# VectorE's inverse root of the next batch moved behind two steps on v, in a three-stage fp32 kernel

## The chip, the cores and the metric

One core of a Trainium2 chip. The metric is the device time of one execution in microseconds: the median was 791.29 over three runs (790.93 to 792.1). The profile is one further execution, of 791.45 us.

## The reference

Batch 8, sequence S = 576, width 512, inner width 1024. Three stages follow each other (einsum and matmul in fp32):

```python
kv  = einsum('bhsd,bhse->bhde', k, v);  out = einsum('bhsd,bhde->bhse', q, kv)
x   = out / sqrt(mean(out * out, -1) + 1e-6) * g_norm          # stage 1: attention, norm
h   = maximum(x @ w_in, 0);  u, v = h[..., :512], h[..., 512:]
v_n = (v - mean(v)) / sqrt(var(v) + 1e-6)                      # stage 2: along the last axis
x   = (u * (w_spatial @ v_n + b_spatial)) @ w_out
h   = maximum(x @ moe2_w_in, 0)                                # stage 3
out = (h * sigmoid(conv3(h))) @ moe2_w_out                     # conv3: three taps along S
```

## The kernel before, in words

Every matrix product of fp32 data is made of three products of parts: an operand is split into a high part (rounded by ScalarE) and a low part (the difference, by VectorE), and high-high, high-low and low-high are summed. This holds for x, for v and for the weights. The product w_out @ moe2_w_in is formed once at the start, so that stage 3 takes the gated values themselves.

**First half (up to about 409 us).** TensorE, ScalarE and VectorE each run body(b) for the 8 batches. Batch b does stage 2 and, for all but the last batch ("ahead"), the attention of batch b + 1. Each engine's order of instructions is written out by hand; engines meet only through counting semaphores (wait_ge). Batches 0 to 2 are unrolled on ScalarE and VectorE, the others run in a loop.

TensorE's order in body(b): kv_product(b + 1) (L404); v_product for the tiles of v (L477), in the order of V_TILES = [0, 1, 2, 4, 3], so that the fifth position is tile 3 and the fourth position is the rest of 64 rows; between them the attention products of b + 1; square_sum(b + 1) (L430), which sums squares over each head; u_product in four parts (L451, 96 matmuls); spatial_product in four parts (L451, 112 matmuls). spatial_product(b, 0) waits for s_vlo to reach 5 (b + 1), that is, for all five v_lo of this batch, and for the first relu of u. kv_product of the next batch waits for `s_g >= b * MT - 1` with the new b and MT = 4: three of the four gates of the batch before.

VectorE's order in body(b): kv_copy(b + 1); then for each position i of the five: v_stats (L1090 to L1097: mean and variance), at the fifth position mean_square(b + 1) (L1041) and inverse_root(b + 1) (L1051 to L1059: one reciprocal and one Newton step on 128 x 144 elements); v_lo of the position before (L1119, for the rest L1121); v_normalise (L1103 to L1112: a reciprocal and a Newton step on one element per row, then the scaling of the tile). After the loop: in batch 0 the low part of the bias row (L1141), v_lo of the fifth position, in batches 1 and 2 the low part of half of w_out2 (L1084), gate(0) (L1126), x_scale(b + 1) four times (L1071), gate(1), x_lo(b + 1) four times (L1076) and once for the rest (L1079), gate(2), gate(3), and four differences of gated blocks (L1174).

ScalarE, in turn, does the relus (L715, L718, L720 for v; L744 for u), the high parts of v (L731; L733 and L734 for the rest), the roots (L694 for r, L725 for v), squares and copies. In batch 0 it also splits w_sp (L853), whose low parts GpSimd forms (L391, L394). In batches 1 and 2 it loads half of w_out2 (L804) and stores its split form to HBM (L812).

SyncE's queue carries most DMAs. In its loop for b: the loads of k, v and q of batch b + 2; spread_r(b + 1), which waits for s_r (set by L1059), stores r0 to HBM in four DMAs (L253), waits for them, and loads it back, each row to 64 partitions, in two DMAs (L258) into rB, called sq_then_r in the profile. x_scale waits for both. Then store_gated(b), which waits for the gates.

**Second half.** Stage 3, batch by batch; nothing of it is touched.

Of the kernel before, what the change touches and what calls it, by code (L numbers as in the profile page):

```python
# [80 lines left out]
def build(nc, q_T, kv_main_dram, kv_rest_dram, consts, w_in, w_sp_T, b_sp, w_out_T, w_in2, w_out2, wo2_dram, op_dram, r_dram, out):  # L81
    with ExitStack() as ctx:
# [940 lines left out]
        def _(dve):  # L1023
# [3 lines left out]
            def kv_copy(a):  # L1027
                dve.wait_ge(s_kv, a + 1)
                dve.wait_ge(s_o, a * MT)
                for half in (0, 1):  # L1030
                    last = dve.tensor_copy(kvd[half * D:(half + 1) * D, :, 1, :],
                                           PS[D:P, KV_BANK, 0:MT * D].rearrange("p (m e) -> p m e", m=MT))
                last.then_inc(s_kvd1, 1)
# [5 lines left out]
            def mean_square(a):  # L1039
                dve.wait_ge(s_ssq, a + 1)  # L1040
                dve.tensor_scalar(ms[:, :], PS[:, ssq_bank(a), 0:QS], 1.0 / D, EPS,  # L1041
                                  ALU.mult, ALU.add).then_inc(s_ms, 1)

            def inverse_root(a):

                dve.wait_ge(s_std, a + 1)
                if isinstance(a, int) and a == 1:
                    dve.wait_ge(s_rP, MT)
                if not isinstance(a, int) or a > 1:
                    dve.wait_ge(s_rst, (a - 1) * 4 * DMA)  # L1050
                dve.reciprocal(r0[:, :], std[:, :]).then_inc(s_nr, 1)  # L1051
                dve.wait_ge(s_nr, a * 4 + 1)
                dve.tensor_tensor(std[:, :], r0[:, :], r0[:, :], ALU.mult).then_inc(s_nr, 1)
                dve.wait_ge(s_nr, a * 4 + 2)
                dve.tensor_tensor(std[:, :], std[:, :], ms[:, :], ALU.mult).then_inc(s_nr, 1)
                dve.wait_ge(s_nr, a * 4 + 3)
                dve.tensor_scalar(std[:, :], std[:, :], -0.5, 1.5, ALU.mult, ALU.add).then_inc(s_nr, 1)
                dve.wait_ge(s_nr, a * 4 + 4)
                dve.tensor_tensor(r0[:, :], r0[:, :], std[:, :], ALU.mult).then_inc(s_r, 1)  # L1059
# [22 lines left out]
            def wo2_low(h, f):  # L1082
                dve.wait_ge(s_wo2_hi, h * MT + f + 1)
                dve.tensor_tensor(wo2_lo[:, f, :], wo2_raw[:, f, :], wo2_hi[:, f, :].bitcast(F32), ALU.subtract).then_inc(s_wo2, 1)  # L1084

            def v_stats(b, p):
                n = P if V_TILES[p] < FULL else REST
                if n == REST:
                    dve.wait_ge(s_vtmp, b + 1)
                    dve.tensor_tensor(v_sb[p % 2][0:n, :], PS[0:n, V_BANK[FULL], 0:F1], v_rest, ALU.add).then_inc(s_vsum, 1)  # L1090
                dve.wait_ge(s_vr, b * NT + p + 1)
                dve.bn_stats(stats[0:n, :], v_sb[p % 2][0:n, :]).then_inc(s_vst, 1)  # L1092
                dve.wait_ge(s_vst, (b * NT + p) * 2 + 1)
                dve.tensor_copy(carrier[0:n, :], stats[0:n, 1:2])
                dve.bn_aggr(mv[0:n, :], stats[0:n, :]).then_inc(s_vst, 1)
                dve.wait_ge(s_vst, (b * NT + p) * 2 + 2)
                dve.tensor_scalar(ve[0:n, :], mv[0:n, 1:2], EPS, None, ALU.add).then_inc(s_ve, 1)  # L1097

            def v_normalise(b, p):
                n = P if V_TILES[p] < FULL else REST  # L1100
                c = (b * NT + p) * 4
                dve.wait_ge(s_vsd, b * NT + p + 1)
                dve.reciprocal(vr0[0:n, :], vsd[0:n, :]).then_inc(s_vrs, 1)  # L1103
                dve.wait_ge(s_vrs, c + 1)
                dve.scalar_tensor_tensor(out=vrr[0:n, :], in0=vr0[0:n, :], scalar=ve[0:n, :], in1=vr0[0:n, :],  # L1105
                                         op0=ALU.mult, op1=ALU.mult).then_inc(s_vrs, 1)
                dve.wait_ge(s_vrs, c + 2)
                dve.tensor_scalar(vrf[0:n, :], vrr[0:n, :], -0.5, 1.5, ALU.mult, ALU.add).then_inc(s_vrs, 1)
                dve.wait_ge(s_vrs, c + 3)
                dve.tensor_tensor(vrs[0:n, :], vr0[0:n, :], vrf[0:n, :], ALU.mult).then_inc(s_vrs, 1)  # L1110
                dve.wait_ge(s_vrs, c + 4)
                dve.tensor_scalar(v_sb[p % 2][0:n, :], v_sb[p % 2][0:n, :], mv[0:n, 0:1], vrs[0:n, :],  # L1112
                                  ALU.subtract, ALU.mult).then_inc(s_vn, 1)

            def v_lo(b, p):
                i, v = V_TILES[p], v_sb[p % 2]
                dve.wait_ge(s_vhi, b * NT + p + 1)
                if i < FULL:
                    dve.tensor_tensor(vn[:, LO, i, :], v, vn[:, HI, i, :].bitcast(F32), ALU.subtract).then_inc(s_vlo, 1)  # L1119
                else:  # L1120
                    dve.tensor_tensor(vnA[REST:P, :], v[0:REST, :], vnA[0:REST, :].bitcast(F32), ALU.subtract).then_inc(s_vlo, 1)  # L1121

            def gate(b, m):
                dve.wait_ge(s_ur, b * MT + m + 1)
                dve.wait_ge(s_sp, b * MT + m + 1)
                dve.tensor_tensor(whole(u_sb[m]), pair[GATE_PAIR[m]], whole(u_sb[m]), ALU.mult).then_inc(s_g, 1)  # L1126

            def body(b, ahead):
                if ahead:
                    kv_copy(b + 1)  # L1130
                for i in range(NT):
                    v_stats(b, i)
                    if ahead and i == NT - 1:
                        mean_square(b + 1)
                        inverse_root(b + 1)
                    if i:
                        v_lo(b, i - 1)
                    v_normalise(b, i)
                if isinstance(b, int) and b == 0:
                    dve.wait_ge(s_b_hi, 1)  # L1140
                    dve.tensor_tensor(wspB[96:97, :], b_raw[96:97, :], wspB[96:97, :].bitcast(F32),  # L1141
                                      ALU.subtract).then_inc(s_b, 1)
                v_lo(b, NT - 1)
                if isinstance(b, int) and b in (1, 2):
                    for f in range(MT):
                        wo2_low(b - 1, f)
                if not ahead:
                    combine_weights()
                gate(b, 0)
                if ahead:  # L1150
                    for m in range(MT):
                        x_scale(b + 1, m)
                gate(b, 1)
                if ahead:
                    for m in range(MT):
                        x_lo(b + 1, m)
                else:
                    for k in range(3):
                        operand_lo(0, k)
                gate(b, 2)  # L1160
                if not ahead:
                    operand_lo(0, 3)
                    operand_lo(0, 4)
                gate(b, 3)
                if ahead:
                    t_a(b)
                    t_b(b)
                    t_c(b)
                else:
                    operand_lo(0, 5)  # L1170
                    operand_lo(0, 6)
# [4 lines left out]
            def t_a(b):  # L1176
                dve.wait_ge(s_To, DMA * b)
                dve.wait_ge(s_g, b * MT + MT)
                t_block(T1, gated(0, 1), gated(0, 0))
                t_block(T3, gated(1, 1), gated(0, 1))  # L1180
# [14 lines left out]
            def combine_weights():  # L1195
                a11, a21, a12, a22 = W[:, 0, 0], W[:, 0, 1], W[:, 1, 0], W[:, 1, 1]
                dve.wait_ge(s_To, DMA * (B - 1))
                dve.tensor_tensor(s_raw[0], a21, a22, ALU.add).then_inc(s_S, 1)
                dve.wait_ge(s_S, 1)
                dve.tensor_tensor(s_raw[1], s_raw[0], a11, ALU.subtract).then_inc(s_S, 1)  # L1200
                weight_lo(S1, 1)
                weight_lo(S2, 2)
                dve.wait_ge(s_Slo, 1)
                dve.tensor_tensor(s_raw[0], a12, s_raw[1], ALU.subtract).then_inc(s_S, 1)
                dve.wait_ge(s_Slo, 2)
                dve.wait_ge(s_S, 3)
                dve.tensor_tensor(s_raw[1], a11, a21, ALU.subtract).then_inc(s_S, 1)
                weight_lo(S4, 3)
                weight_lo(S3, 4)
                weight_lo(A11, 5)  # L1210
                weight_lo(A12, 6)
                weight_lo(A22, 7)
# [240 lines left out]
```

## Time and profile before

| | |
|---|---|
| median of three runs | 791.29 us (790.93 to 792.1) |
| the profiled execution | 791.45 us, its span 789.4 us |
| granted TensorE clock | 1.00 over the span |
| busy: TensorE | 780.9 us (99%) |
| busy: VectorE | 584.9 us (74%) |
| busy: ScalarE | 421.6 us (53%) |
| busy: GpSimd | 29.5 us (4%) |
| GpSimd's last instruction | from 65.96 to 67.45 us |

In the profile PE is TensorE's matmul, PEld its weight load, DVE VectorE, ACT ScalarE, POOL GpSimd and SP SyncE; SPq and ACTq are the DMA issues of a queue. L1059 is line 1059 of the kernel. A wait for several semaphores is put down to whatever ended last, which need not be the one that the code names.

### The profile page before, as it was taken

The numbers are of one execution on the slowest core, as the hardware profiler recorded it, in microseconds if no ns is written. First come the engines' busy times: TensorE is split into PE (matmuls) and PEld (weight loads), VectorE is DVE, ScalarE is ACT, GpSimd is POOL, SyncE is SP. The second block draws the span as 40 slices with busy tenths as digits, with TensorE's granted clock in tenths as the row PEclk, the third lists the DMA queues.
The fourth block names the chain that finished last, engine by engine and source line by source line (L and its number), as shares of the span: only waits on it lengthen the run. The fifth ranks groups of instructions, "written<-read, shape, count | busy, mean of one in ns | idle before, by whom it ended". The sixth has DMA issues, their size and how long they took to land.

```text
span 789.4 us, 15393 instructions
## 1 busy us (share of the span) xinstructions
PE 780.9 (99%) x5654; PEld 701.4 (89%) x5654; DVE 584.9 (74%) x1262; ACT 421.6 (53%) x753; POOL 29.5 (4%) x40
## 2 busy tenths in 40 slices
PE   8999999999999999999999999999999999999997
PEld 7679889797988979899999898998989899898986
DVE  3766786776577475666899989497985979679791
ACT  4664462634335253352557767365774757567562
POOL 4342000000000000000000000000000000000000
PEclk9999999999999999999999999999999999999999
DMA  9872455756334272222192212221021312102102
GB/s 329 301 253 62 172 196 185 293 182 234 96 110 174 75 269 61 105 52 77 39 360 67 103 54 106 67 96 64 4 104 65 105 53 94 64 13 105 53 0 66
DMA packets 35001, 96.86 MB, mean 123 GB/s; under 512 B 2738, under 2 KB 9106, under 8 KB 30228
## 3 DMA queue, kind: packets, MB, share of 16 engines
q1 hardware_dynamic: 33476, 90.09, 33.3%
q10 hardware_dynamic: 1488, 6.30, 2.1%
q8 instruction: 20, 0.33, 0.2%
q14 instruction: 17, 0.14, 0.1%
HBM read 66.11 MB, written 30.28 MB: 122 GB/s over the span
## 4 chain that ended last, share of the span: by engine, by line
PE 93%; DVE 3%; DMA 1%; ACT 1%; issue 1%; SPq 1%; ACTq 0%; DVEq 0%
PE ps L451 27%; PE ps L634 25%; PE ps L626 21%; PE ps L477 11%; PE ps L420 2%; PE ps L404 2%; PE ps L484 2%; PE ps L556 1%; DMA work<-w_out_T_dram 1%; PE ps L430 1%; DVE h_and_sums L1272 0%; DVE vrr L1105 0%; DVE t_then_s L1174 0%; PE ps L544 0%; DVE work L1112 0%
## 5 line engine op out<-in xcount | busy, mean ns | idle before, releaser
L634 PE MATMUL ps<-w_in_split,v_hg_split 128*128 128x512 f32 x832 | 194.9, 389 | 0.0
L634 PEld LDWEIGHTS ps<-w_in_split,v_hg_split 128*128 128x128 f32 x832 | 155.7, 188 | 32.3
L451 PE MATMUL ps<-w_sp_split,v_hg_split 128*128 128x288 f32 x896 | 120.2, 295 | 1.7 <-ACT work L744 1.7
L451 PEld LDWEIGHTS ps<-w_sp_split,v_hg_split 128*128 128x128 f32 x896 | 119.2, 188 | 1.9 <-issue 1.9
L451 PE MATMUL ps<-x_operand_split,w_in_split 128*128 128x288 f32 x768 | 103.8, 295 | 0.0
L451 PEld LDWEIGHTS ps<-x_operand_split,w_in_split 128*128 128x128 f32 x768 | 102.0, 188 | 1.7 <-issue 1.6
L477 PE MATMUL ps<-w_in_split,x_operand_split 128*128 128x512 f32 x384 | 92.8, 394 | 0.0
L477 PEld LDWEIGHTS ps<-w_in_split,x_operand_split 128*128 128x128 f32 x384 | 70.9, 188 | 18.2 <-issue 3.1
L1272 DVE TENSOR_TENSOR h_and_sums<-h_and_sums,ps 128x288 f32<-128x288 f32 x160 | 68.8, 453 | 7.5 <-PE ps L626 7.2
L1126 DVE TENSOR_TENSOR work<-ps,work 128x576 f32<-128x576 f32 x32 | 24.1, 757 | 61.2 <-PE ps L451 60.9
L1272 DVE TENSOR_TENSOR h_and_sums<-work,ps 128x288 f32<-128x288 f32 x64 | 28.3, 452 | 46.8 <-PE ps L626 46.3
L626 PE MATMUL ps<-x_operand_split,w_combined 128*128 128x288 f32 x384 | 61.5, 295 | 0.0
L915 ACT ACTIVATE h_and_sums<-h_and_sums 128x576 f32<-128x576 f32 x64 | 43.4, 678 | 29.3 <-DVE h_and_sums L1272 28.3
L626 PE MATMUL ps<-operand_more_split,w_combined_more 128*128 128x288 f32 x384 | 56.5, 295 | 0.3 <-DVE h_and_sums L1272 0.3
L626 PEld LDWEIGHTS ps<-x_operand_split,w_combined 128*128 128x128 f32 x384 | 54.7, 188 | 0.0
L626 PEld LDWEIGHTS ps<-operand_more_split,w_combined_more 128*128 128x128 f32 x384 | 52.9, 188 | 0.6 <-DVE h_and_sums L1272 0.6
L1315 DVE SCALAR_TENSOR_TENSOR work<-h_and_sums,const_cols,work 128x576 f32<-128x576 f32 x64 | 52.5, 821 | 0.3
L1309 DVE SCALAR_TENSOR_TENSOR work<-h_and_sums,const_cols,work 128x576 f32<-128x576 f32 x64 | 52.5, 820 | 0.0
L921 ACT ACTIVATE work<-h_and_sums,const_cols 128x576 f32<-128x576 f32 x64 | 49.7, 776 | 3.0
L1320 DVE TENSOR_TENSOR work<-h_and_sums,work 128x576 f32<-128x576 f32 x64 | 48.7, 761 | 0.3 <-ACT work L931 0.3
L1092 DVE BATCH_NORM_STATS2 bn_stats<-work 128x6 f32<-128x512 f32 (+1 forms) x40 | 27.5, 688 | 24.1 <-ACT work L715 18.5
L931 ACT ACTIVATE work<-work 128x576 f32<-128x576 f32 x64 | 43.6, 681 | 2.3 <-DVE work L1315 1.8
(124 smaller groups left out, 1037.5 us busy)
## 6 DMA issues: line engine op xcount, KB each, us to landing
kv_raw<-kv_main_dram SPq DMA_DIRECT2D x8, 2048.0 KB, 10.1
q_raw<-q_T_dram SPq DMA_DIRECT2D x8, 1152.0 KB, 7.2
operand_scratch<-t_then_s SPq DMA_DIRECT2D x8, 1152.0 KB, 5.3
operand_raw<-operand_scratch SPq DMA_DIRECT2D x8, 1152.0 KB, 5.5
sq_then_r<-r_scratch SPq DMA_DIRECT2D x14, 576.0 KB, 6.1
operand_scratch<-work SPq DMA_DIRECT2D x24, 288.0 KB, 2.6
operand_more_raw<-operand_scratch SPq DMA_DIRECT2D x8, 864.0 KB, 7.4
w_out_split_scratch<-v_hg_split ACTq DMA_DIRECT2D x2, 2048.0 KB, 8.4
```

The source lines that it names most:

```text
L451: last = pe.matmul(pair[bank][:, c, :], st, mo[:, c * HALF:(c + 1) * HALF], start=(n == 0), stop=(n == len(steps) - 1))
L477: last = pe.matmul(PS[:, V_BANK[i], 0:F1], XG[:, a, m, i * P:(i + 1) * P], WA[:, w, m, F1:2 * F1], start=(n == 0), stop=(n == len(steps) - 1))
L626: last = pe.matmul(PS[:, n % 8, 0:HALF], st, mo, start=(i == 0), stop=(i == len(steps) - 1))
L634: last = pe.matmul(PS[:, ROW_BANK[i], :], x, wout2[:, w, F_ORDER[e], :], start=(e == 0 and n == 0), stop=(e == FT - 1 and n == len(PASSES) ...
L915: act.activation(h_sb[f][:, 1:S + 1], h_sb[f][:, 1:S + 1], ACT.Relu).then_inc(s_hr, 1)
L921: act.activation(t_sb[e % 2], h_sb[f][:, 1:S + 1], ACT.Copy, scale=cols[:, FT + f:FT + f + 1]).then_inc(s_t0, 1)
L931: act.activation(p_sb[e % 2], t_sb[e % 2], ACT.Sigmoid).then_inc(s_sig, 1)
L1092: dve.bn_stats(stats[0:n, :], v_sb[p % 2][0:n, :]).then_inc(s_vst, 1)
L1272: dve.tensor_tensor(dst, x, PS[:, (g * NPROD + k) % 8, 0:HALF], ALU.add).then_inc(s_sum, 1)
L1309: dve.scalar_tensor_tensor(out=t, in0=h_sb[f][:, 0:S], scalar=cols[:, f:f + 1], in1=t, op0=ALU.mult, op1=ALU.add).then_inc(s_cv1, 1)
L1315: dve.scalar_tensor_tensor(out=t, in0=h_sb[f][:, 2:S + 2], scalar=cols[:, 2 * FT + f:2 * FT + f + 1], in1=t, op0=ALU.mult, op1=ALU.add).th ...
L1320: dve.tensor_tensor(p_sb[e % 2], h_sb[F_ORDER[e]][:, 1:S + 1], p_sb[e % 2], ALU.mult).then_inc(s_mul, 1)
```

## The change

On VectorE, in the loop over the five positions, mean_square(b + 1) stays where it is, and inverse_root(b + 1) moves behind the loop, that is, behind v_lo of the fourth position and v_normalise of the fifth. In batch 0 it stands ahead of L1141, in all of them ahead of v_lo of the fifth position.

```diff
                     v_stats(b, i)
                     if ahead and i == NT - 1:
                         mean_square(b + 1)
-                        inverse_root(b + 1)
                     if i:
                         v_lo(b, i - 1)
                     v_normalise(b, i)
+                if ahead:
+                    inverse_root(b + 1)
                 if isinstance(b, int) and b == 0:
                     dve.wait_ge(s_b_hi, 1)
```

## Rows read from the trace of the kernel before

**Rows 1.** The page: busy us (share of the span) and instructions of each engine.

```profile
PE 780.9 (99%) x5654; PEld 701.4 (89%) x5654; DVE 584.9 (74%) x1262; ACT 421.6 (53%) x753; POOL 29.5 (4%) x40
```

**Rows 2.** Timeline of VectorE, end of batch 0: start, duration, instruction [idle before <- releaser].

```profile
62.26 0.30 DVE L1041 TENSOR_SCALAR ms<-ps 128x144 f32<-128x144 f32 x1
63.28 1.05 DVE L1051 RECIPROCAL r<-std 128x144 f32<-128x144 f32 x1 [0.72 <-ACT std L694]
...
64.75 1.42 DVE L1055 TENSOR_TENSOR std<-std,ms 128x144 f32<-128x144 f32 x1
66.19 1.35 DVE L1057 TENSOR_SCALAR std<-std 128x144 f32<-128x144 f32 x1
67.58 0.31 DVE L1059 TENSOR_TENSOR r<-r,std 128x144 f32<-128x144 f32 x1
...
69.47 0.55 DVE L1112 TENSOR_SCALAR work<-work,mean_var,vrs 128x512 f32<-128x512 f32 x1
70.05 0.76 DVE L1141 TENSOR_TENSOR w_sp_split<-w_sp_raw,w_sp_split 1x576 fp32r<-1x576 f32 x1
70.84 0.69 DVE L1119 TENSOR_TENSOR v_hg_split<-work,v_hg_split 128x512 fp32r<-128x512 f32 x1
```

**Rows 3.** Timeline of ScalarE and of GpSimd, the same stretch.

```profile
61.84 0.62 ACT L734 ACTIVATE v_hg_split<-work 64x512 fp32r<-64x512 f32 x1
...
63.15 0.19 ACT L725 ACTIVATE vsd<-ve 128x1 f32<-128x1 f32 x1
...
63.11 1.44 POOL L391 TENSOR_TENSOR w_sp_split<-w_sp_raw,w_sp_split 128x576 fp32r<-128x576 f32 x1 [2.80 <-ACT w_sp_split L853]
64.53 1.47 POOL L391 TENSOR_TENSOR w_sp_split<-w_sp_raw,w_sp_split 128x576 fp32r<-128x576 f32 x1
65.96 1.49 POOL L394 TENSOR_TENSOR w_sp_split<-w_sp_raw,w_sp_split 64x576 fp32r<-64x576 f32 x1
```

**Rows 4.** Timeline of VectorE and of GpSimd, 58 to 60 us.

```profile
59.13 1.20 DVE L1105 SCALAR_TENSOR_TENSOR vrr<-vr,ve 64x1 f32<-64x1 f32 x1
...
58.43 1.88 POOL L391 TENSOR_TENSOR w_sp_split<-w_sp_raw,w_sp_split 128x576 fp32r<-128x576 f32 x1 [3.54 <-ACT w_sp_split L853]
```

**Rows 5.** Timeline of TensorE and VectorE, 71 to 89 us.

```profile
71.79 15.09 PE L451 MATMUL ps<-w_sp_split,v_hg_split 128*128 128x288 f32 x112 [1.67 <-ACT work L744]
86.81 2.55 PE L404 MATMUL ps<-kv_raw 128*64 128x64 f32 x80
...
78.54 3.01 DVE L1071 SCALAR_TENSOR_TENSOR o_x<-o_x,const_cols,sq_then_r 128x576 f32<-128x576 f32 x4 [1.93 <-DMA sq_then_r<-r_scratch]
...
85.13 0.75 DVE L1126 TENSOR_TENSOR work<-ps,work 128x576 f32<-128x576 f32 x1
```

**Rows 6.** The same in batch 1, 109 to 136 us.

```profile
109.86 1.05 DVE L1051 RECIPROCAL r<-std 128x144 f32<-128x144 f32 x1 [0.39 <-ACT std L694]
...
111.90 0.31 DVE L1059 TENSOR_TENSOR r<-r,std 128x144 f32<-128x144 f32 x1
...
123.57 3.00 DVE L1071 SCALAR_TENSOR_TENSOR o_x<-o_x,const_cols,sq_then_r 128x576 f32<-128x576 f32 x4
...
130.32 0.76 DVE L1126 TENSOR_TENSOR work<-ps,work 128x576 f32<-128x576 f32 x1
...
133.85 2.55 PE L404 MATMUL ps<-kv_raw 128*64 128x64 f32 x80
```

**Rows 7.** The store's issue; then queues' packets, MB, share: 121 to 121.5, 104 to 106.

```profile
119.11 0.35 ACTq L812 DMA_DIRECT2D w_out_split_scratch<-v_hg_split  x1
...
q10 hardware_dynamic: 8, 0.13, 81.7%
q1 hardware_dynamic: 13, 0.05, 46.3%
...
q1 hardware_dynamic: 81, 0.71, 86.7%
q10 hardware_dynamic: 85, 0.14, 20.7%
```

## The prediction, made before the change was run

> **What bounds the kernel now.** I read the page's busy shares first: TensorE is busy for 780.9 of 789.4 us [rows 1], so the change can only matter where TensorE waits, or where it could begin to. Next the chain of waits in order of time. It runs over TensorE nearly without a break from 72 us to the end of the first stage (409 us), but from 51 to 71.8 us it runs over VectorE. So I looked at TensorE's own timeline: before the spatial product of batch 0 it stands still for 1.67 us, up to 71.79 [rows 5]. The profile names ScalarE's L744 as releaser. By the code that product waits for the first relu only, which ended long before, and for all five s_vlo, the last from VectorE's L1119, which ends at 71.53 [rows 2]. So VectorE is the cause, and TensorE resumes 0.26 us behind it. Batches 1 to 6 have no such wait, and batch 7 does not pass through the moved call. What the change can win is therefore at most 1.67 us; what it can lose has to be looked for behind the thing that it delays, r.
>
> **The change, part by part.**
>
> *Nothing is added or removed; five instructions move.* inverse_root(b + 1) (L1051 to L1059) goes behind v_lo of position 3 and v_normalise of position 4. It does not go behind v_lo of position 4, the one that TensorE waits for. VectorE still issues all of it, and L1141 too, before that last v_lo. So the text of the change doesn't shorten the list of work ahead of the critical instruction; it can gain only the idle time that the order fills. That is 0.72 us before L1051, the wait for the root [rows 2].
>
> *Batch 0, up to r.* L1041 ends at 62.56 [rows 2]. v_lo(3) has its input at 62.46 [rows 3], so it runs from 62.59 to 63.28 (0.69, as L1119 in rows 2). The root of the variance is there at 63.34 [rows 3], so v_normalise(4) starts at 63.38. Undisturbed, v_lo(3) and v_normalise(4) take 2.13 us together (67.89 to 70.02 in rows 2), 1.4 for the latter. But now it meets GpSimd, whose three operations lie back to back from 63.11 to 67.45 [rows 3]. In the trace those hold VectorE up: L1055 takes 1.42 and ends 0.17 after the second, L1057 takes 1.35 and ends 0.09 after the third [rows 2, 3]; undisturbed the whole inverse root takes 2.35 (109.86 to 112.21 in rows 6), here 4.61. L1105, an instruction of v_normalise on one element, was held in the same way at 59.13: 1.20 us, until GpSimd's end at 60.31 [rows 4]. So the stall isn't a property of the inverse root, and moves onto what takes its place: L1103 (it reads a single tensor, as L1051, which ran beside GpSimd in its usual 1.05) ends at 63.54; L1105 is held to 64.57; L1108 is free, to 64.76; L1110 is held to 66.02; L1112 is held to 67.45 and then needs 0.40 more (its 0.55 less the 0.15 that L1057 saved of its own by having been queued), to 67.85. Then the inverse root runs undisturbed, 2.35: r is there at 70.23 instead of 67.89, **2.34 later**. L1141 (0.76) and the last v_lo (0.69) follow, to 71.74 instead of 71.53: **TensorE resumes 0.21 later**, and the 0.72 is not won. Bounds for this step: if nothing of v_normalise is held, it ends at 64.8, the inverse root meets the third GpSimd operation once and r comes at 68.23 (+0.34); the last v_lo then ends at 69.7 and the whole 1.67 goes. If L1108 is held too, everything is 0.2 later. I take the middle case, since rows 4 show the very instruction held and rows 2 the two kinds that follow.
>
> *Batch 0, behind r.* SyncE's queue waits for r, stores it (four DMAs), waits for them and loads rB (two DMAs); no other call is moved past, and store_gated behind it in that queue waits for later gates anyway. From r to rB it is 10.61 us: 67.89 to 78.50, where VectorE's L1071 has stood idle for the DMA for 1.93 us already [rows 5]. That wait has no cover left, so the 2.34 go straight through. On VectorE, in order, behind L1071 are gate(1), x_lo, gate(2). gate(2), the L1126 at 85.13, ends at 85.88; it will end at 88.22. TensorE's kv_product of the next batch waits for that gate (s_g of 4b - 1). It started at 86.81 [rows 5], with 0.93 to spare. The new start is 88.22 and a hand-over of 0.04 to 0.26 (the latter as at 71.53 to 71.79); with 0.15 it is 88.37, **1.5 us later than before** (this contains the 0.21, which disappears into the wait). ScalarE's x_hi moves along and has slack.
>
> *Batches 1 to 6.* GpSimd is done by then. The idle 0.39 before L1051 [rows 6] is filled; v_lo(3) and v_normalise(4) end at 109.50 + 2.13 = 111.63, the inverse root at 114.0 instead of 112.21: r is 1.8 later. The last v_lo, at 115.04 before, comes some 1 us earlier, which is worth nothing: TensorE starts the spatial product at 118.9 without a wait. rB lands 10.61 after r, at 122.8 before, 0.75 ahead of L1071 at 123.57, which gate(0) holds; now at 124.6, which delays L1071 by 1.05. gate(2) (130.32, 0.76) ends at 132.1, and TensorE wants it at 133.85 [rows 6]: 1.7 us of slack left, no cost. That pattern repeats about 47 us apart six times.
>
> *But batches 1 and 2 have a second transfer.* ScalarE issues the 2 MB store of w_out at 119.11 (and 47 us later), bound by TensorE, not by what is moved; its packets start at 121 us just as those of rB, some 5 us of them, run out [rows 7]. Shifted by 1.8, the last 2.1 us of them fall beside the store. Where two queues had work at 104 to 106 us, they took 81 and 85 packets [rows 7], one for one. rB has packets of 9.2 KB (0.66 us each), the store of 16 KB (0.62), so rB's rest stretches from 2.1 to 4.1 us: rB lands at 126.7, L1071 starts 3.1 later, gate(2) ends at 134.2, and TensorE's kv_product, wanted at 133.85, starts at about 134.35: **0.5 us in each of the two batches**. Bounds: 0 (no stretch beyond 1.6 us) and 4.4 (rB's rest stands still until the store is through, 6 us). The Trainium skill ("DMA: Bandwidth & Descriptors", section "Queues, rings and completion order") says that an engine changes queues only behind a packet of some 9 to 17 descriptors. Each engine has about 8 entries of rB, so by that rule the rest could go out first and the 0.5 be nearly 0; the row of 104 us speaks for the even split, and I keep the 0.5 in the sum.
>
> *Sum.* Executions of the profile: 791.45 (span 789.4 and 2.05 around it) + 1.5 + 2 x 0.5 = 793.95. That execution lies 0.16 above the median of 791.29, so on the scale of the medians it is **793.8**, 0.3% slower.
>
> **Rivals.**
>
> *A, the store takes nothing.* Only the first wait, at 88 us, appears: 791.29 + 1.5 = 792.8. For it: the overlap needs rB's last packets to be slowed by more than 1.6 us before TensorE notices, and before the change the two touch without any visible harm. Against: the even split at 104 us. The Trainium skill's rule on packets, above, would make this case the likelier one.
>
> *B, not slower: v_normalise isn't held by GpSimd.* Place: L1105 to L1112 at 63.5 us. Then the last v_lo ends at 69.7, TensorE goes from 70.12 straight on (-1.67), r is 0.34 late, gate(2) ends at 86.22 and kv_product starts at 86.4 instead of 86.81: 791.29 - 0.4 = 790.9. It decides as soon as r is less than about 0.8 late and the store costs nothing. For it: L1110 and L1112 are nowhere seen beside a GpSimd operation. Against: rows 4, and that L1055 and L1057 are of their kinds. Even here the gate takes back three quarters of the gain.
>
> *C, the store starves rB.* 4.4 us in each of two batches: 791.3 + 1.5 + 8.8 = 801.6. For it: where the two meet now, from 121 to 121.5 us, the store has 81.7% of the engines' time and rB 46.3% [rows 7]. Against: rB had little left to do then.
>
> *D, the gate isn't what kv_product waits for, or rB comes sooner when it starts later.* Then only the 0.21 stands: 791.5. Against: the wait is in the code, and nothing else moves data between 72 and 77 us, so the load has no reason to be quicker.
>
> **Chances and range.** Forecast 0.45, A 0.23, B 0.13, C 0.04, D 0.15. A measurement of this kernel can tell about 0.2%, 1.6 us, from no change. The forecast and C are slower by that; A lies at 1.5 and is split evenly; D counts as the same; B lies within it, with a part of 0.05 where the full 1.67 is kept. Less a little of the forecast (a hand-over at its short end and a milder overlap) this gives slower 0.57, same 0.38, faster 0.05. Range: 791.0 to 795.5, which takes in D, A and overlaps of up to 1.4 us a batch, and leaves out C and most of B; the forecast's own range is 792.9 to 795.0.
>
> **What would show it.** In batch 0: L1105, L1110 and L1112 of the fifth position long (1.0, 1.2, 1.7) and L1055, L1057 at 0.3 and 0.2; r near 70.2; the spatial product at 72.0; L1071 at about 80.8; a new idle time of TensorE before L404 of about 1.2 us near 88 us. In batches 1 and 2: L1071 idle for rB until some 3 us behind its gate, and a second and third idle time of TensorE before L404, about 0.5 each. In batches 3 to 6: L1071 about 1 us later against its gate and no idle TensorE. I am wrong if v_normalise keeps its 1.4 us in batch 0, or if kv_product starts before gate(2) has ended.

## The result

The changed kernel takes 793.3 us (median of 16 runs, 792.49 to 793.87), the kernel before 791.62 beside it (16 runs): a ratio of 1.0021, with a 95% interval of 1.0014 to 1.0027. That is 1.1 to 2.1 us slower. The forecast was 793.8.

Columns as in the rows of before. First the page's busy shares, which answer to [rows 1] and hide everything:

```profile
PE 781.2 (99%) x5654; PEld 701.8 (89%) x5654; DVE 584.1 (74%) x1262; ACT 421.0 (53%) x753; POOL 29.5 (4%) x40
```

Then the waits of TensorE in the trace of after: engine, line, what it waited for: us in total, times, longest. The second is new.

```profile
PE ps L451 <- DVE v_hg_split L1119: 1.5, 1, 1.5
PE ps L404 <- DVE work L1126: 1.3, 1, 1.3
```

This profiled execution reached batch 0 later than that of before, because a weight load at the start landed 0.5 us later: L404 of batch 0 starts at 38.48 instead of 37.91. So 0.57 is to be taken off its times before they are set against those of before. The timelines of VectorE, GpSimd and TensorE, for [rows 2, 3, 5]:

```profile
63.13 0.68 DVE L1121 TENSOR_TENSOR v_hg_split<-work,v_hg_split 64x512 fp32r<-64x512 f32 x1
...
64.11 1.01 DVE L1105 SCALAR_TENSOR_TENSOR vrr<-vr,ve 128x1 f32<-128x1 f32 x1
...
65.35 1.17 DVE L1110 TENSOR_TENSOR vrs<-vr,vrf 128x1 f32<-128x1 f32 x1
66.56 1.61 DVE L1112 TENSOR_SCALAR work<-work,mean_var,vrs 128x512 f32<-128x512 f32 x1
68.09 1.04 DVE L1051 RECIPROCAL r<-std 128x144 f32<-128x144 f32 x1
...
69.51 0.31 DVE L1055 TENSOR_TENSOR std<-std,ms 128x144 f32<-128x144 f32 x1
69.85 0.24 DVE L1057 TENSOR_SCALAR std<-std 128x144 f32<-128x144 f32 x1
70.12 0.31 DVE L1059 TENSOR_TENSOR r<-r,std 128x144 f32<-128x144 f32 x1
...
71.25 0.69 DVE L1119 TENSOR_TENSOR v_hg_split<-work,v_hg_split 128x512 fp32r<-128x512 f32 x1
...
81.12 3.01 DVE L1071 SCALAR_TENSOR_TENSOR o_x<-o_x,const_cols,sq_then_r 128x576 f32<-128x576 f32 x4 [4.11 <-DMA sq_then_r<-r_scratch]
...
87.71 1.42 DVE L1126 TENSOR_TENSOR work<-ps,work 128x576 f32<-128x576 f32 x2
...
63.66 2.85 POOL L391 TENSOR_TENSOR w_sp_split<-w_sp_raw,w_sp_split 128x576 fp32r<-128x576 f32 x2 [2.79 <-ACT w_sp_split L853]
66.46 1.43 POOL L394 TENSOR_TENSOR w_sp_split<-w_sp_raw,w_sp_split 64x576 fp32r<-64x576 f32 x1
...
72.20 15.08 PE L451 MATMUL ps<-w_sp_split,v_hg_split 128*128 128x288 f32 x112 [1.52 <-DVE v_hg_split L1119]
88.61 2.55 PE L404 MATMUL ps<-kv_raw 128*64 128x64 f32 x80 [1.33 <-DVE work L1126]
```

What GpSimd holds has changed sides: the long instructions are now L1105, L1110 and L1112 of v_normalise, while L1055 and L1057 have their short times. r is ready at 70.43, or 69.86 on the clock of before, where it was 67.89: 1.97 late. L1071 follows 10.7 us behind it and gate(2), the first of the two L1126 at 87.71, ends near 88.5. TensorE has stood still since 87.3 and starts L404 at 88.61. The spatial product starts at 71.63 on the clock of before, where it was 71.79: the moved root won next to nothing there.

In batch 1 (for [rows 6]) L1071 waits for rB too, and TensorE doesn't notice:

```profile
115.29 0.31 DVE L1059 TENSOR_TENSOR r<-r,std 128x144 f32<-128x144 f32 x1
...
126.56 3.01 DVE L1071 SCALAR_TENSOR_TENSOR o_x<-o_x,const_cols,sq_then_r 128x576 f32<-128x576 f32 x4 [1.16 <-DMA sq_then_r<-r_scratch]
...
133.15 0.75 DVE L1126 TENSOR_TENSOR work<-ps,work 128x576 f32<-128x576 f32 x1
...
135.59 2.55 PE L404 MATMUL ps<-kv_raw 128*64 128x64 f32 x80
```

gate(2) ends 1.7 us before L404. And rB, r to L1071, took 10.96 us, 0.31 more than in batch 0 before (67.89 to 78.54), although the store of w_out had been issued at 120.86. The DMA queues (packets, MB, share) of 123.5 to 124 us and then of 124 to 125 us, for [rows 7], show why:

```profile
q1 hardware_dynamic: 14, 0.13, 121.3%
...
q1 hardware_dynamic: 22, 0.18, 90.0%
q10 hardware_dynamic: 2, 0.03, 10.2%
```

Queue 1 (rB) kept the engines to its end, and the store (queue 10) waited: it landed 10.0 and 11.2 us after its issue in the two batches instead of 8.4, and nobody waits for it.

### The profile page after: what moved, and what is told of

Read it like the earlier page. It is cut to its first block, busy times and chain, and to the rows that moved or that the text cites. A ratio compares the mean times of both kernels' runs of the same rounds, so it can differ in the third digit from the quotient of the medians.

```text
span 791.1 us, 15393 instructions
## 1 busy us (share of the span) xinstructions
PE 781.2 (99%) x5654; PEld 701.8 (89%) x5654; DVE 584.1 (74%) x1262; ACT 421.0 (53%) x753; POOL 29.5 (4%) x40
## 4 chain that ended last, share of the span: by engine, by line
PE 91%; DVE 3%; DMA 2%; ACT 1%; issue 1%; SPq 1%; ACTq 0%; DVEq 0%
PE ps L634 25%; PE ps L451 25%; PE ps L626 21%; PE ps L477 11%; PE ps L420 2%; PE ps L404 2%; PE ps L484 2%; PE ps L556 1%; DMA work<-w_out_T_dram 1%; PE ps L430 1%; DMA sq_then_r<-r_scratch 1%; DVE vrr L1105 0%; DVE h_and_sums L1273 0%; DVE t_then_s L1175 0%; PE ps L544 0%
## 5 line engine op out<-in xcount | busy, mean ns | idle before, releaser
L477 PE MATMUL ps<-w_in_split,x_operand_split 128*128 128x512 f32 x384 | 92.8, 394 | 0.0
L477 PEld LDWEIGHTS ps<-w_in_split,x_operand_split 128*128 128x128 f32 x384 | 71.0, 188 | 18.1 <-issue 3.1
L1126 DVE TENSOR_TENSOR work<-ps,work 128x576 f32<-128x576 f32 x32 | 24.0, 754 | 61.5 <-PE ps L451 61.5
L1321 DVE TENSOR_TENSOR work<-h_and_sums,work 128x576 f32<-128x576 f32 x64 | 48.1, 752 | 0.3 <-ACT work L931 0.3
L700 ACT ACTIVATE x_operand_split<-o_x 128x576 fp32r<-128x576 f32 x32 | 22.0, 687 | 48.1 <-DVE o_x L1071 44.7
## 6 DMA issues: line engine op xcount, KB each, us to landing
w_out_split_scratch<-v_hg_split ACTq DMA_DIRECT2D x2, 2048.0 KB, 10.6
```

Of the source, the lines that this page charges most:

```text
L477: last = pe.matmul(PS[:, V_BANK[i], 0:F1], XG[:, a, m, i * P:(i + 1) * P], WA[:, w, m, F1:2 * F1], start=(n == 0), stop=(n == len(steps) - 1))
L1321: dve.tensor_tensor(p_sb[e % 2], h_sb[F_ORDER[e]][:, 1:S + 1], p_sb[e % 2], ALU.mult).then_inc(s_mul, 1)
```

## The experiments

L404 of batch 0 starts anywhere from 37.67 to 38.91 us in the twelve traces, a scatter nearly as large as the effect. A measure that doesn't contain it is the distance from L404 of batch 0 to L404 of batch 1. All of the change's effect shows itself there: from L404 of batch 1 to that of batch 6 it is 235.11 us in the trace of before and 235.05 in that of after. It is 48.90 us in the trace of before and 50.13 in that of after, 1.23 more. The table gives it beside the medians (all runs of a line on one chip).

| kernel | median, us | before beside it | ratio (95%) | L404 to L404, against before |
|---|---|---|---|---|
| only0 | 792.96 | 791.47 | 1.0017 (1.0008 to 1.0026) | +1.38 |
| not0 | 791.59 | 791.47 | 0.9999 (0.9990 to 1.0008) | -0.01 |
| gate2_first | 792.47 | 791.47 | 1.0009 (1.0000 to 1.0018) | -0.16, then +0.87 to the L404 after that |
| root_last | 816.64 | 791.47 | 1.0322 (1.0306 to 1.0337) | +2.69 |
| before_free | 790.12 | 791.87 | 0.9978 (0.9967 to 0.9988) | -1.92 |
| after_free | 789.98 | 791.87 | 0.9979 (0.9970 to 0.9988) | -1.69 |
| before_early | 790.46 | 791.87 | 0.9980 (0.9971 to 0.9989) | -0.39 |
| after_early | 791.95 | 791.87 | 1.0001 (0.9992 to 1.0010) | -0.33 |
| before_early_again | 790.55 | 791.66 | 0.9987 (0.9978 to 0.9996) | +0.78 |
| spread_split | 791.29 | 791.66 | 0.9995 (0.9986 to 1.0004) | -0.23 |

**only0 and not0: in which batch is the price?** The diff of only0 against before; not0 has `late` the other way round.

```diff
+                late = isinstance(b, int) and b == 0
...
                         mean_square(b + 1)
-                        inverse_root(b + 1)
+                        if not late:
+                            inverse_root(b + 1)
...
+                if ahead and late:
+                    inverse_root(b + 1)
```

> The moved inverse root in batch 0 alone, the old order in batches 1 to 6. Theory (the whole price is the wait of kv_product for gate(2) at 88 us, made by r being late in batch 0 and rB landing without cover): the same time as the changed kernel, 1.2 to 1.7 us over the kernel before, with 1.3 us of idle TensorE before L404 near 88 us. Rival (part of the price is spread over batches 1 to 6: the store of w_out, or the later rB): clearly less than the changed kernel, by 0.3 us or more.

> The moved inverse root in batches 1 to 6, the old order in batch 0. Theory: no difference to the kernel before (within 0.2 us), since gate(2) still ends 1.7 us ahead of kv_product although rB lands some 2 us later; the store of w_out lands later (10.6 us instead of 8.4) and nobody waits for it. Rival (the later r costs something in every batch): 0.3 us or more over the kernel before.

Measured: 1.5 us over before for only0, 0.1 for not0, whose interval of +-0.7 us alone would hide a part of the rival's price; its distance in the trace, equal to that of before, doesn't. only0's trace has the new wait:

```profile
PE ps L404 <- DVE work L1126: 1.5, 1, 1.5
```

The price stands in batch 0, in that wait.

**gate2_first: is it gate(2) that kv_product waits for?** Against after:

```diff
                 gate(b, 1)
+                if isinstance(b, int) and b == 0:
+                    gate(b, 2)
...
-                gate(b, 2)
+                if not (isinstance(b, int) and b == 0):
+                    gate(b, 2)
```

> The changed kernel, and in batch 0 gate(2) directly behind gate(1), ahead of the four x_lo. Theory: gate(2) ends near 85.5 us, kv_product starts without a wait, and the 1.3 us go: within 0.3 us of the kernel before (the spatial product starts 0.1 us earlier than there). x_lo ends near 89 us, when v_product wants it at 89.7. Rival (kv_product waits for something else that came later, such as the k and v loads): still 1 us or more over the kernel before, with the idle time before L404.

Measured: the wait before L404 is gone and L404 comes 0.16 earlier than before. But the median is 1.0 us over before, outside what I had written down. The next distance, to the L404 after that, is 47.91 us where it was 47.04. The wait of TensorE that lies in it, and VectorE's timeline:

```profile
PE ps L477 <- DVE kv_double L1031: 0.7, 1, 0.7
...
92.49 0.87 DVE L1031 COPY kv_double<-ps 64x256 f32<-64x256 f32 x2
```

gate(3) and the four differences of gated blocks stand behind x_lo and are late as well; kv_copy is queued behind them, and the attention product of the next batch, asked for in the last matmul of v_product, waits for it. So the mechanism is confirmed, and the remedy buys less than half: over the two distances 0.7 us of the 1.2 are left, by the medians 1.0 of 1.7. A list that runs 2 us late is late for its next customer.

**root_last: what a later r costs when its cover is used up.** Against after:

```diff
-                if ahead:
-                    inverse_root(b + 1)
...
                 v_lo(b, NT - 1)
+                if ahead:
+                    inverse_root(b + 1)
```

> The changed kernel with the inverse root behind the last v_lo as well, in all batches. Theory: the spatial product of batch 0 starts without a wait (1.5 us won), but r is late by 3.5 us against the kernel before in batch 0 and by 4.9 in batches 1 to 6, against a cover of 0.9 us at gate(2) in batch 0 and 3.4 in the others (of which 0.75 lies ahead of L1071): kv_product waits 4.3 us in batch 0 and about 1.4 in each of the six others, in all 2.8 + 8.4 = 11 us over the kernel before, some 803. Rival (only the last v_lo matters, r has cover everywhere but in batch 0): about 2.8 us over the kernel before.

Measured: 25 us slower, more than twice what I expected. The parts that I had worked out came out right: no wait before the spatial product; in batch 0 a wait of 4.5 us before L404 (4.3 expected), in batches 3 to 5 of 1.39, 1.31 and 1.24 (1.4 expected). Two things were missing. In batches 1 and 2 the wait is 6.3 and 6.0 us, since this time the store comes first. VectorE's timeline and the queues from 124 to 125, 126 to 128 and 128 to 130 us:

```profile
120.64 0.31 DVE L1059 TENSOR_TENSOR r<-r,std 128x144 f32<-128x144 f32 x1
...
136.73 3.01 DVE L1071 SCALAR_TENSOR_TENSOR o_x<-o_x,const_cols,sq_then_r 128x576 f32<-128x576 f32 x4 [9.03 <-DMA sq_then_r<-r_scratch]
...
q10 hardware_dynamic: 31, 0.51, 119.7%
...
q10 hardware_dynamic: 48, 0.79, 105.0%
...
q10 hardware_dynamic: 32, 0.52, 100.9%
q1 hardware_dynamic: 16, 0.15, 17.4%
```

rB, issued at 123.8, moves nothing before 129.0, when the store (issued at 123.4) is nearly through, and lands 15.8 us behind r instead of 10.7. And behind the long waits TensorE runs slowly. Its timeline, then busy times by stretch (PE, PEld, DVE, ACT, POOL; then the granted clock, DMA share, GB/s):

```profile
89.40 4.05 PE L404 MATMUL ps<-kv_raw 128*64 128x64 f32 x80 [4.53 <-DVE work L1126]
...
90.00:91.00 1.00, 1.00 (x27) 1.00 (x24) 0.97 (x2) 0.00 (x0) 0.00 (x0) 0.51 0.00 0
...
94.00:96.00 2.00, 2.00 (x10) 1.66 (x9) 0.36 (x1) 0.26 (x1) 0.00 (x0) 1.00 1.00 376
```

The 80 matmuls of kv_product take 4.05 us instead of 2.55, at a granted clock of 0.51, the lower level of 1.2 GHz. After the two waits of 6 us they take 4.27 and 4.20; after those of 1.2 to 1.4 us the clock stays up and they take 2.55. Together: 20.7 us of waits before L404, 1.0 before L477 in batch 6, 4.9 of slow matmuls, less the wait of 1.7 before the spatial product, makes 24.9 of the 25.2 measured.

**before_free and after_free: is it GpSimd that makes VectorE late?** Both leave out the low parts of w_sp for j = 2, 3 and 4 but for 8 columns (j = 4 by the same slice in a branch that is not shown) and fill the rest with zeros, in two operations from 46.5 to 48.1 us:

```diff
+                t = slice(0, S) if j < 2 else slice(0, 8)
                 if j < FULL:
-                    pool.tensor_tensor(wsp[:, LO, j, :], sp_raw[:, j, :], ...
+                    pool.tensor_tensor(wsp[:, LO, j, t], sp_raw[:, j, t], ...
```

> The kernel before, with GpSimd's last three operations (the low parts of w_sp for j = 2, 3, 4) on 8 of 576 columns; the rest of those low parts is filled with zeros at about 46 us, so this leaves out part of the computation. Theory (GpSimd holds VectorE for some 2.2 us between 63 and 67.5 us, whatever stands there): L1055 and L1057 take 0.3 and 0.2 us, r is there 2.2 us earlier, the last v_lo ends before TensorE needs it, the wait at 71 us goes: 1.4 to 1.7 us faster than the kernel before, 789.9. Rival (the long L1055 and L1057 have another cause): no change.

> The changed kernel with the same thing left out. Theory: v_normalise takes 1.4 us instead of 4.2, r comes 0.7 us ahead of the kernel before, both waits of TensorE (before the spatial product and before kv_product) go but for 0.2 us: also 1.4 to 1.7 us faster than the kernel before, and within 0.4 us of before_free. So the order costs nothing once GpSimd is out of the way. Rival (the order itself is what costs): at least 1 us slower than before_free.

Measured: 1.75 and 1.89 us under before, 0.1 apart; I had expected 1.4 to 1.7. after_free's line numbers are 4 higher; its L1109, L1114, L1116 and L1059 are L1105, L1110, L1112 and L1055 of before:

```profile
63.44 0.22 DVE L1109 SCALAR_TENSOR_TENSOR vrr<-vr,ve 128x1 f32<-128x1 f32 x1
...
63.88 0.16 DVE L1114 TENSOR_TENSOR vrs<-vr,vrf 128x1 f32<-128x1 f32 x1
64.08 0.55 DVE L1116 TENSOR_SCALAR work<-work,mean_var,vrs 128x512 f32<-128x512 f32 x1
...
65.97 0.31 DVE L1059 TENSOR_TENSOR std<-std,ms 128x144 f32<-128x144 f32 x1
...
PE ps L408 <- DVE work L1130: 0.2, 1, 0.2
```

None of these is held, and of both waits of TensorE 0.2 us is left. The two orders are then worth the same. In before_free TensorE starts the spatial product 12.82 us behind the first product of u, in before 14.65 us: what stood to be won was 1.83 us, not the 1.67 that the idle column shows.

**before_early, after_early: a complete kernel with less of GpSimd's work there.** ScalarE's splits of w_sp, for which GpSimd waits, are moved ahead in batch 0. Those for j = 1, 2 and 3 stand two positions earlier, that for j = 0 behind the root of position 0 instead of in position 2, and that for j = 4 stays:

```diff
-                    if first and i >= 2:
-                        sp_hi(i - 2)
+                    if first and i in (1, 2, 3):
+                        sp_hi(i)
...
                     v_root(b, i)
+                    if first and i == 0:
+                        sp_hi(0)
...
-                    sp_hi(3)
                     sp_hi(4)
```

> The kernel before, with ScalarE's splits of w_sp in batch 0 one position earlier (nothing left out), so that only one GpSimd operation is left behind 63 us. Theory: L1057 alone is held, r comes 1.5 us earlier, the wait before the spatial product shrinks from 1.7 to some 0.2 us: 1.2 to 1.5 us faster than the kernel before, 790.2, the fastest complete kernel so far. Rival (the earlier splits delay ScalarE's copies and hold VectorE in positions 1 and 2 instead, and the chain of VectorE passes it on): less than 0.5 us faster.

> The changed kernel with the same earlier splits. Theory: v_normalise(4) is through before the one remaining GpSimd operation, the inverse root meets it once, r comes 0.7 us ahead of the kernel before, no wait before the spatial product and at most 0.2 us before kv_product: 1.3 to 1.6 us faster than the kernel before, level with before_early. Rival (the order costs by itself): 1 us slower than before_early.

> The same kernel as before_early, once more. Its median was 1.4 us under the kernel before, but its profiled execution was one of the slowest (791.57), and there ScalarE's first split of w_sp waited for the load of w_sp and moved every later step of batch 0 by about 1 us. If that was one late load: the median again 1.2 to 1.6 us under the kernel before, and in this trace POOL's first L391 starts some 8.2 us behind L404 of batch 0 (9.4 in the other), with a TensorE wait of 0.2 to 0.5 us before the spatial product. If the load is late as a rule: a median less than 0.6 us under the kernel before and the same wait of 1.2 us.

Measured: before_early is 1.4 us under before, and 1.1 when run again, both intervals below one. It is the fastest complete kernel here, and it has the old order. after_early is level with before: I had expected the one GpSimd operation left (64.29 us here) to meet the inverse root. But the earlier splits cost VectorE some 0.2 us ahead of that point (L1098 of the fifth position starts 24.5 us behind L404 of batch 0, in before, as L1097, 24.3), so its last step of v_normalise (L1113, the L1112 of before) began just then and was held for 1.2 us, and r was late again. VectorE's timeline and TensorE's waits in after_early:

```profile
64.24 1.76 DVE L1113 TENSOR_SCALAR work<-work,mean_var,vrs 128x512 f32<-128x512 f32 x1
...
PE ps L404 <- DVE work L1127: 1.2, 1, 1.2
```

The traces of before_early don't show its gain. The second median, 1.1 us under, lies just short of the 1.2 to 1.6 expected for one late load and well beyond the 0.6 for a load that is late as a rule, so neither case came out as written. Both profiled executions, 791.57 and 791.89 us, are among the slowest of their kernel; in both, ScalarE's first split came late and the relu and statistics of position 1 with it. The second, where I had looked for a start some 8.2 us behind L404 of batch 0, has GpSimd's first L391 at 10.6, 48.26 against 37.67, and TensorE waits 1.2 us before the spatial product. Eight of the 11 timed executions of each set are under 790.7. That the faster ones find the load of w_sp landed in time is plausible, but none was traced. after_early's trace, with the same splits, has it in time (the first split starts without a wait, GpSimd's first L391 8.3 us behind L404 of batch 0), and that execution, 790.88, is the fastest of its 11.

**spread_split: do the holds ahead of 63 us count too?** The same kernel with the first three splits one position later, at 1, 2 and 3, and the fourth behind the root of position 3:

```diff
-                    if first and i >= 2:
-                        sp_hi(i - 2)
+                    if first and i in (1, 2, 3):
+                        sp_hi(i - 1)
...
                     v_root(b, i)
+                    if first and i == 3:
+                        sp_hi(3)
...
-                    sp_hi(3)
                     sp_hi(4)
```

> The kernel before, with ScalarE's splits of w_sp placed otherwise: the first behind v_hi(0), the fourth behind the root of position 3, so that no split can meet a late load. GpSimd's operations then start near 49.3, 53.5, 58.4, 60.3 and 64.5 us. Theory (what counts is which VectorE instructions stand beside GpSimd, wherever that is): it holds L1105 of position 1 for 0.7 us and L1110 or L1112 of position 3 for about 1 us, which the chain passes on, and wins 1.1 us behind 63 us: within 0.7 us of the kernel before, no gain like before_early. Rival (only the holds behind 63 us matter): 1.2 us faster or more.

Measured: 0.4 us under before, within the interval. In its trace L1106 of position 1 and L1111 of position 3 (L1105 and L1110 of before) are held. In before they took 0.22 and 0.15 us:

```profile
50.78 1.18 DVE L1106 SCALAR_TENSOR_TENSOR vrr<-vr,ve 128x1 f32<-128x1 f32 x1
...
61.54 1.18 DVE L1111 TENSOR_TENSOR vrs<-vr,vrf 64x1 f32<-64x1 f32 x1
```

What it wins behind 63 us it has paid ahead of it.

## Why the prediction was right, and where not

*The ceiling and the cause of the wait.* Right: VectorE's last v_lo released the spatial product, not ScalarE's L744 that the profile named; after's trace now names L1119.

*The hold moves onto v_normalise.* Right, instruction by instruction: L1105, L1110 and L1112 took 1.01, 1.17 and 1.61 us, L1108 was free. The sizes: r was 1.97 late where 2.34 had been worked out. GpSimd's last operation ended 0.13 earlier, L1112 needed 0.28 behind it instead of 0.40, and the inverse root began 0.08 before L1112's end instead of 0.03 behind it: 0.36 together. For the same reason the spatial product started 0.16 earlier instead of 0.21 later. before_free and after_free show that the hold is what made the order matter in batch 0.

*r to kv_product.* Right: 10.7 us from r to L1071 with no cover, the wait at gate(2) of 1.33 us, and 1.23 us of distance lost in the trace (1.38 in only0), where 1.5 had been forecast. only0, not0 and gate2_first place it there and nowhere else.

*Batches 3 to 6.* Right: L1071 waits 0.95 to 1.08 us for rB in batches 3 to 5, 0.54 in batch 6, and TensorE doesn't wait. root_last confirms the size of the cover, to 0.2 us.

*The store in batches 1 and 2.* Wrong: 0.5 us each was forecast, none came, and L1071 waited 1.16 and 0.87 us for rB, where some 3 had been given as the sign. The failed step is "rB's rest stretches from 2.1 to 4.1 us", read off two queues that had taken 81 and 85 packets from 104 to 106 us. That row never showed a sharing. The same view of the kernel before, from 104 to 104.5 and from 104.5 to 106 us:

```profile
q10 hardware_dynamic: 78, 0.13, 76.9%
q1 hardware_dynamic: 16, 0.13, 63.8%
...
q1 hardware_dynamic: 65, 0.58, 94.4%
q10 hardware_dynamic: 7, 0.01, 2.0%
```

Queue 10 was running out while queue 1 began: two transfers behind each other, which the longer window averages into an even split. In after the rB load was there first and was not shared with, so the mechanism of rival A was the case. The traces agree in both directions with the rule that stood against my row, that of the Trainium skill (DMA: Bandwidth & Descriptors, "Queues, rings and completion order"), by which an engine changes queues only behind a packet of some 9 to 17 descriptors. rB's 128 rows are 8 for each of the 16 engines, and rB went out whole in after, the store in root_last.

*The sum.* Without the store it is 1.5 us. The medians say 1.7 with 1.1 to 2.1, only0 says 1.5 with 0.6 to 2.1, the trace 1.2. These agree within their scatter; whether 0.3 us lies anywhere beside the one wait can't be told. The forecast of 793.8 stands 0.5 over the measured 793.3, but part of that nearness is luck. It was counted from a median of 791.29 over three runs, and over 16 the kernel before takes 791.62. As a difference 2.5 us were forecast and 1.7 measured, 0.8 too much, by a term of 1.0 that wasn't there. Rival A's 1.5 is the nearer one.

## What to carry to other kernels

Before moving an instruction ahead of another, list who waits for the one that is pushed back: here a root that seemed to delay TensorE's next product by 1.7 us fed a chain of two DMAs (10.7 us) whose cover was already zero, and the price came 17 us later, at another wait. An instruction with a long duration in one place of a trace may be held by a neighbour engine; then moving it only changes who is held, and the thing to move is the neighbour's work. A remedy that undoes one wait should be checked for the next user of the same late list.

## What was not expected of the hardware

Two large transfers on different queues did not share the engines: whichever had its packets there first went out whole. A load of 10.7 us took 10.96 with a 2 MB store issued behind it and 15.8 with the store ahead of it. VectorE's instructions on a single element per row (L1105, L1110) took up to 1.2 us beside GpSimd's, where 0.2 is usual, while its reciprocals kept their usual time there (L1051 1.05 us, L1103 0.16). And the three waits of TensorE of 4.5 to 6.3 us cost a second time, 1.5 to 1.7 us each of matmuls at a granted clock near 0.5, which those of 1.2 to 1.4 us did not.
